# One tile loop for the last two experts of a mixture-of-experts stage, in plain fp32

## The chip, the cores and the metric

The program runs on one core of one Trainium2 chip. The metric is the device time of one execution in microseconds; lower is better. The engines are named as in the profile: PE (TensorE, matrix products; PEld is its weight load), ACT (ScalarE), DVE (VectorE), POOL (GpSimd) and SP (SyncE, which here issues most of the DMAs). PEldq, ACTq and the like are the sequencers of the engines.

## What is computed

Three stages in a row. Block-causal attention (4 batches, 8 heads, 576 rows, 64 columns a head) gives 2304 tokens of 512 columns. A dense layer with 2048 hidden columns and a leaky maximum follows. Then a layer of 8 experts with top-1 routing, around which this case turns:

```python
skip_score = x @ w_skip
do_compute = skip_score > 0
out = x.copy()
xc = x[do_compute]
logits = xc @ w_gate
e_idx = np.argmax(logits, axis=1)
...
for e in range(E):                      # E = 8
    mask = e_idx == e
    if not mask.any():
        continue
    h = np.maximum(xc[mask] @ w1[e], 0.0)      # 512 -> 1024
    y[mask] = gate_w[mask, None] * (h @ w2[e]) # 1024 -> 512
out[do_compute] = xc + y
```

All inputs and outputs are fp32. How many tokens an expert gets depends on the data.

## The kernel before

**The first two stages** (attention, the dense layer's two products in three passes of fp32r each) fill PE until about 610 us and aren't touched, but for one constant: POOL writes a set of tables at the start of the dense layer's second product, each counted by the semaphore `s_tables` (N_TABLES, 20, L470).

**Tiles of the experts.** The tokens of each expert are put in tiles of 128 rows. DVE counts them (L1447 to L1459): the count of each expert plus `fill`, which is 128 (L883), shifted right by 7 bits. Every expert thus has at least one tile, which may be partly or wholly empty. A sum over the experts gives the first tile of each, `base_i`, which every engine loads into registers (`tile_start`, L577; a register load from a tensor, with the register operations after it). One full tile of expert 0, the early tile, is taken from the first tokens already known and is worked through ahead of the loops in straight code, with a second product in plain fp32 (`early_hidden` L1777, `early_y` L1796).

**Eight loops.** PE, ACT and DVE each have eight loops, one for each expert, from that expert's first tile to the next one's; POOL has one over all tiles (L956). What PE does for a tile (L1850 to L1873):

- the first product, 32 products of 128x128 by 128x128 in fp32 (L1859), into the two banks `ps_hid`;
- four transposes of the next tile's rows (L1786);
- the second product, 24 products of 512 columns in fp32r (L1870 to L1872): high by high, high by low and low by high parts, into `ps_y`.

ACT copies the rows (`held`, L1121, then `kept`, L1151), and takes the rectified high part of the hidden values out of `ps_hid` (L1154). DVE takes the low part (L1483), moves the transposed rows (L1463) and multiplies the result by the gate weight and adds the row (L1490). POOL gathers the rows of the tile after next (L941) and scatters the result to the output (L933), both with indirect DMAs.

**Weights.** SP loads 4 MB an expert in eight pieces into four sets of buffers (`w1_sb`, `w2_sb`, `load_expert` L698), expert x into set x mod 4, once the expert four before is done. At the head of an expert's loop, ACT splits off the high part of w2, four pieces of 1024 columns (`high_w2`, L1130), once the last expert's second product is done, since there is one `w2_hi`; DVE makes the low part in place of w2 (`low_w2`, L1468).

Of the kernel before, what the change touches and what calls it, by code (L numbers as in the profile page):

```python
# [7 lines left out]
F32 = mybir.dt.float32  # L8
F32R = mybir.dt.float32r
BF16 = mybir.dt.bfloat16  # L10
I32 = mybir.dt.int32
ALU = mybir.AluOpType
ACT = mybir.ActivationFunctionType
AX = mybir.AxisListType

P = 128
B, H, S, D = 4, 8, 576, 64
N_TOK = B * S
DM = H * D
# [65 lines left out]
MAX_TILES = NT + E  # L85
SKIP = float(1 << 20)
NW = 4


EARLY_BLK = 4  # L90
# [128 lines left out]
def build(nc, q_t, k_t, v_r, w_in, w_out, w_gs, w1, w2, out):  # L219
    ctx = ExitStack()  # L220
    with ctx:
        def sb(name, shape, dt=F32, scope=ctx):
            return scope.enter_context(nc.sbuf_tensor(name, shape, dt))
# [4 lines left out]
        def sem(name):  # L228
            return ctx.enter_context(nc.semaphore(name))
# [106 lines left out]
        sb("gap", [P, max(pad - used, 0) // 4 // 16 * 16 + 16])  # L336


        w1_sb += [sb(f"w1_sb{i}", [P, KC, F]) for i in range(2, NW)]
        w2_sb += [sb(f"w2_sb{i}", [P, EC, DM], F32, raw) for i in range(2, NW)]  # L340
        raw.close()
        w2_lo += [sb(f"w2_lo{i}", [P, EC, DM], F32R) for i in range(2, NW)]
        idx = sb("idx", [P, E * SLOTS], I32)
        below = sb("below", [P, E + 1, E])
        rows = sb("rows", [P, ROW_W])
        held = sb("held", [P, ROW_W])
        kept = sb("kept", [P, ROW_W])
# [86 lines left out]
        s_rank = sem("s_rank")  # L434
        s_tab = sem("s_tab")
        s_cnt = sem("s_cnt")
        s_t = sem("s_t")
        s_early = sem("s_early")
        s_earlyat = sem("s_earlyat")
# [27 lines left out]
        block = ctx.enter_context(nc.Block())  # L467

        N_FULL, N_CONST, N_GAP = 3, 12, 6
        N_TABLES = 20  # L470
        W_LOADS = KC + EC // 2


# [82 lines left out]
        def loaded_to(e, x, n):  # L556

            for k, loaded in enumerate(s_w[x % NW]):
                e.wait_ge(loaded, 16 * (W_LOADS // 2 * (x // NW) + (n + 2 - k) // 2))

        def tab_of(m):

# [69 lines left out]
        def _(e):  # L632
# [133 lines left out]
            for x in range(2, E):  # L766
                if x >= NW:
                    e.wait_ge(s_expert, x - NW + 1)
                    e.wait_ge(s_w2lo, W2_PIECES * (x - NW + 1))
                for n in range(W_LOADS):  # L770
                    load_expert(x, n)
            e.wait_ge(s_count, 1)
            total_tiles = e.value_load(base_i[0:1, E:E + 1], min_val=0, max_val=MAX_TILES)
            for i in range(2):
# [6 lines left out]
        def _(e):  # L781
# [103 lines left out]
            for c in range(KC):  # L885
# [7 lines left out]
            e.tensor_copy(rev[:, :], rev_i[:, :]).then_inc(s_tables, 1)  # L893
            e.affine_select(out=lower[:, :, :], in_=lower[:, :, :], compare_op=ALU.is_gt, fill=0.0,
                            base=0, pattern=[[1, E + 1], [-1, E]], channel_multiplier=0).then_inc(s_tables, 1)


            for ring in range(ACT_RING):
# [71 lines left out]
        def _(e):  # L970
# [148 lines left out]
            def hold(g):  # L1119
                e.wait_ge(m_gather, (g + 1) * 16)  # L1120
                e.copy(held[:, :], rows[:, :]).then_inc(m_held, 1)  # L1121
# [20 lines left out]
            early_relu(1)  # L1142
            starts = tile_starts(e)
            hold(0)
            for x in range(E):
                for n in range(W2_PIECES):
                    high_w2(x, n)
                with e.Fori(starts[x], starts[x + 1]) as g:
                    e.wait_ge(m_held, g + 1)
                    e.wait_ge(m_out, g + 1)  # L1150
                    e.copy(kept[:, :], held[:, :]).then_inc(m_kept, 1)  # L1151
                    for half in range(2):
                        e.wait_ge(m_hid, 2 * g + half + 2)
                        e.activation(hid_hi[:, EC // 2 * half:EC // 2 * (half + 1), :].rearrange("p f c -> p (f c)"),  # L1154
                                     ps_hid[half][:, :], ACT.Relu).then_inc(m_high, 1)
                    e.wait_ge(m_kept, g + 2)
                    hold(g + 1)


        @block.vector  # L1160
        def _(e):
# [296 lines left out]
            e.wait_ge(s_t, 5)  # L1458
            e.tensor_copy(base_i[:, :], base_f[:, :]).then_inc(s_count, 1)  # L1459

            def move_rows_t(g):
                e.wait_ge(m_rt, g + 1)
                e.tensor_copy(rows_t[:, :, :].rearrange("p k c -> p (k c)"), ps_rt[:, :]).then_inc(m_rows, 1)  # L1463

            def low_w2(x, n):
# [7 lines left out]
            e.wait_ge(m_y, 1)  # L1473
            e.scalar_tensor_tensor(out=y_out[:, :], in0=ps_y[:, :], scalar=early[:, DM:DM + 1],
                                   in1=early[:, 0:DM], op0=ALU.mult, op1=ALU.add).then_inc(m_out, 1)
            for x in range(E):
                for n in range(W2_PIECES):
                    low_w2(x, n)
                with e.Fori(starts[x], starts[x + 1]) as g:
                    for half in range(2):  # L1480
                        fs = slice(EC // 2 * half, EC // 2 * (half + 1))
                        e.wait_ge(m_high, 2 * g + half + 2)
                        e.scalar_tensor_tensor(out=hid_lo[:, fs, :].rearrange("p f c -> p (f c)"), in0=ps_hid[half][:, :],  # L1483
                                               scalar=0.0, in1=hid_hi[:, fs, :].rearrange("p f c -> p (f c)").bitcast(F32),
                                               op0=ALU.max, op1=ALU.subtract).then_inc(m_low, 1)
                    move_rows_t(g + 1)
                    e.wait_ge(m_y, g + 2)
                    e.wait_ge(m_kept, g + 2)
                    e.wait_ge(m_scatter, (g + 1) * 16)
                    e.scalar_tensor_tensor(out=y_out[:, :], in0=ps_y[:, :], scalar=kept[:, DM:DM + 1],  # L1490
                                           in1=kept[:, 0:DM], op0=ALU.mult, op1=ALU.add).then_inc(m_out, 1)


        @block.tensor
        def _(e):
# [351 lines left out]
                starts.append(tile_start(e, f))  # L1847
            starts.append(tile_start(e, E))

            for x in range(E):  # L1850
                i = x % NW
                with e.Fori(starts[x], starts[x + 1]) as g:
                    e.wait_ge(m_rows, g + 1)
                    loaded_to(e, x, KC - 1)
                    e.wait_ge(m_low, 2 * g + 1)
                    for half in range(2):
                        for f in range(EC // 2 * half, EC // 2 * (half + 1)):
                            for c in range(KC):
                                last = e.matmul(ps_hid[half][:, P * f - HALF * half:P * (f + 1) - HALF * half],  # L1859
                                                w1_sb[i][:, c, P * f:P * f + P], rows_t[:, c, :],  # L1860
                                                start=c == 0, stop=c == KC - 1)
                        last.then_inc(m_hid, 1)
                    transpose_rows(g + 1)
                    e.wait_ge(m_out, g + 1)
                    for f in range(EC):
                        if f % 2 == 0:
                            e.wait_ge(s_w2lo, W2_PIECES * x + f // 2 + 1)
                        if f % (EC // 2) == 0:
                            e.wait_ge(m_low, 2 * g + f // (EC // 2) + 2)
                        e.matmul(ps_y[:, :], hid_hi[:, f, :], w2_hi[:, f, :], start=f == 0, stop=False)  # L1870
                        e.matmul(ps_y[:, :], hid_hi[:, f, :], w2_lo[i][:, f, :], start=False, stop=False)  # L1871
                        last = e.matmul(ps_y[:, :], hid_lo[:, f, :], w2_hi[:, f, :], start=False, stop=f == EC - 1)  # L1872
                    last.then_inc(m_y, 1)  # L1873


_NAMES = ("q_t", "k_t", "v_r", "w_in", "w_out", "w_gs", "w1", "w2")
# [24 lines left out]
```

## Time and profile before

| | us |
|---|---|
| median of 3 runs (779.55 to 780.79) | 780.35 |
| the profiled execution, its own time | 779.68 |
| span of its instructions in the trace | 777.9 |
| PE busy in that span | 759.8 |
| DVE, ACT, POOL busy | 371.2, 304.2, 151.1 |

The span goes from the first to the last instruction that the profiler recorded, and the 1.78 us between it and the execution's time lie outside the records. Sums below are made against the profiled execution. In the trace a plain fp32 product leaves two records on PE, an fp32r product leaves one. Matmuls are pipelined, so that the duration of one is longer than its distance from the next: the time that a stretch of them takes is read from the chain of waits, not from a mean.

### The profile page before, as it was taken

To read this page: it belongs to the slowest core of one execution; us is meant where nothing else is said; L and a number is where in the kernel's file an instruction comes from. 1 tells how busy PE (TensorE), PEld (TensorE's weight loads), DVE (VectorE), ACT (ScalarE), POOL (GpSimd) and SP (SyncE) were. 2 spreads that over 40 slices of the span, in tenths; PEclk is the share of its full clock that TensorE was granted. 3 is DMA by queue.
4 is the path that set the end of the run, shared out by engine and by line. 5 is a ranking of instruction groups with operands and counts; after the bars stand their busy time and mean duration, and the time that the engine had idled before them with its cause. 6 is when DMAs were issued, how large, how long until landed. Compare 5 with 4: busy or idle time off the path is not lost.

```text
span 777.9 us, 13549 instructions
## 1 busy us (share of the span) xinstructions
PE 759.8 (98%) x4738; PEld 643.7 (83%) x4738; DVE 371.2 (48%) x772; ACT 304.2 (39%) x711; POOL 151.1 (19%) x193
## 2 busy tenths in 40 slices
PE   7999999999999999999999999999999999999997
PEld 4556888888888887999988888888878779898996
DVE  5767455533433563023254556556463341444644
ACT  5566664544344553334432222213221131333533
POOL 3226664312212331100020000000000031222222
PEclk9999999999999999999999999999999999999999
DMA  4336777544544542466665665655552147777750
GB/s 133 118 112 175 206 202 213 159 110 130 150 110 128 148 117 64 139 179 174 182 198 166 184 177 149 191 165 169 165 165 69 37 131 244 234 241 218 241 160 4
DMA packets 97959, 121.68 MB, mean 156 GB/s; under 512 B 14258, under 2 KB 61122, under 8 KB 97896
## 3 DMA queue, kind: packets, MB, share of 16 engines
q1 hardware_dynamic: 94920, 116.50, 51.5%
q0 software_dynamic: 2080, 3.77, 1.5%
q8 instruction: 36, 0.59, 0.3%
q10 hardware_dynamic: 896, 0.59, 0.2%
q14 instruction: 27, 0.22, 0.1%
HBM read 89.35 MB, written 31.57 MB: 155 GB/s over the span
## 4 chain that ended last, share of the span: by engine, by line
PE 91%; ACT 2%; issue 2%; SPq 2%; DMA 2%; DVE 1%; POOL 0%; POOLq 0%; DVEq 0%; ACTq 0%
PE ps_hid L1859 10%; PE ps_h L1615 9%; PE ps_x L1692 9%; PE ps_x L1694 8%; PE ps_x L1693 8%; PE ps_h L1617 8%; PE ps_h L1616 8%; PE ps_o L1597 5%; PE ps_t L1571 4%; PE ps_y L1871 3%; PE ps_y L1872 3%; PE ps_y L1870 3%; PE ps_s L1558 1%; PE ps_s L1559 1%; PE ps_s L1522 1%
## 5 line engine op out<-in xcount | busy, mean ns | idle before, releaser
L1615 PE MATMUL ps_h<-xh,win_h 128*128 128x384 f32 x384 | 135.2, 352 | 3.0 <-ACT act L1013 2.1
L1617 PE MATMUL ps_h<-xh,win_l 128*128 128x384 f32 x384 | 128.7, 335 | 0.0
L1616 PE MATMUL ps_h<-xl,win_h 128*128 128x384 f32 x384 | 128.7, 335 | 0.0
L1692 PE MATMUL ps_x<-wout_h,g_hi 128*128 128x512 f32 x288 | 114.6, 398 | 0.0
L1694 PE MATMUL ps_x<-wout_h,g_lo 128*128 128x512 f32 x288 | 112.4, 390 | 0.0
L1693 PE MATMUL ps_x<-wout_l,g_hi 128*128 128x512 f32 x288 | 112.2, 389 | 0.0
L1013 ACT ACTIVATE act<-ps_h 128x384 f32<-128x384 f32 x96 | 47.2, 491 | 149.0 <-PE ps_h L1617 148.7
L1194 DVE TENSOR_REDUCE neg_max<-ps_s 128x1 f32<-128x128 f32 (+3 forms) x144 | 71.0, 509 | 48.8 <-PE ps_s L1559 26.5
L999 ACT ACTIVATE prob<-ps_s,neg_max 128x128 f32<-128x128 f32 (+3 forms) x144 | 78.9, 550 | 37.8 <-DVE neg_max L1194 30.6
L1859 PEld LDWEIGHTS ps_hid<-rows_t,w_sb 128*128 128x128 f32 x704 | 80.2, 192 | 1.7 <-issue 0.8
L1615 PEld LDWEIGHTS ps_h<-xh,win_h 128*128 128x128 f32 x384 | 72.1, 188 | 11.6 <-ACT act L1013 5.8
L1234 DVE TENSOR_TENSOR g_lo<-g_raw,g_hi 128x512 fp32r<-128x512 f32 x72 | 49.6, 689 | 65.8 <-ACT g_hi L1023 65.3
L1859 PE MATMUL ps_hid<-rows_t,w_sb 128*128 128x128 f32 x704 | 80.5, 275 | 0.0
L1616 PEld LDWEIGHTS ps_h<-xl,win_h 128*128 128x128 f32 x384 | 72.3, 188 | 0.0
L1617 PEld LDWEIGHTS ps_h<-xh,win_l 128*128 128x128 f32 x384 | 72.1, 188 | 0.0
L1200 DVE COPY pt<-ps_t 128x384 f32<-128x384 f32 (+4 forms) x113 | 46.8, 434 | 51.9 <-PE ps_t L1571 51.6
L1692 PEld LDWEIGHTS ps_x<-wout_h,g_hi 128*128 128x128 f32 x288 | 54.1, 188 | 12.3 <-issue 2.0
L1694 PEld LDWEIGHTS ps_x<-wout_h,g_lo 128*128 128x128 f32 x288 | 54.1, 188 | 11.6
L1693 PEld LDWEIGHTS ps_x<-wout_l,g_hi 128*128 128x128 f32 x288 | 54.1, 188 | 10.4
L1023 ACT ACTIVATE g_hi<-g_raw 128x512 fp32r<-128x512 f32 x72 | 43.8, 630 | 47.1 <-DVE g_raw L1229 31.7
L1229 DVE SCALAR_TENSOR_TENSOR g_raw<-g_raw 128x512 f32<-128x512 f32 x72 | 49.3, 686 | 15.9 <-DMA g_raw<-hidden 15.6
L1571 PE MATMUL ps_t<-ident,prob 128*128 128x128 f32 x339 | 54.8, 278 | 0.9 <-DVE pt L1200 0.7
(187 smaller groups left out, 1064.0 us busy)
## 6 DMA issues: line engine op xcount, KB each, us to landing
w_sb<-in_w SPq DMA_DIRECT2D x64, 512.0 KB, 5.3
hidden<-act SPq DMA_DIRECT2D x96, 192.0 KB, 2.3
g_raw<-hidden SPq DMA_DIRECT2D x72, 256.0 KB, 4.3
k_raw<-in_k_t SPq DMA_DIRECT2D x40, 144.0 KB, 3.0
x2rows<-x SPq DMA_DIRECT2D x18, 256.0 KB, 2.4
out<-x SPq DMA_DIRECT2D x18, 256.0 KB, 2.7
w_stage<-in_w_in SPq DMA_DIRECT2D x16, 256.0 KB, 3.1
w_stage<-in_w_out SPq DMA_DIRECT2D x16, 256.0 KB, 3.0
```

The source lines that it names most:

```text
L999: e.activation(prob_of(u), score_out(u), ACT.Exp, bias=neg_max[:, u % 4:u % 4 + 1], scale=1.0, accum_out=row_sum[p % 2][:, sum_column(u):s ...
L1194: e.tensor_reduce(out=neg_max[:, u % 4:u % 4 + 1], in_=src, axis=AX.XY if u % UNITS == TAIL else AX.X, op=ALU.max, negate=True).then_inc(s ...
L1229: e.scalar_tensor_tensor(out=raw[:, :, :], in0=raw[:, :, :], scalar=0.01, in1=raw[:, :, :], op0=ALU.mult, op1=ALU.max).then_inc(s_leaky, 1)
L1234: e.tensor_tensor(g_lo[j % G_RING][:, :, :], g_raw[j % RAW_RING][:, :, :], g_hi[j % G_RING][:, :, :].bitcast(F32), ALU.subtract).then_inc( ...
L1571: last = e.transpose(t_bank(u, P, P * kt, P * kt + P), tile[:, P * kt:P * kt + P], ident[:, :])
L1615: e.matmul(dst, win_h[:, f, kc, :], xh[slot][:, kc, :], start=kc == 0, stop=False)
L1616: e.matmul(dst, win_h[:, f, kc, :], xl[slot][:, kc, :], start=False, stop=False)
L1617: last = e.matmul(dst, win_l[:, f, kc, :], xh[slot][:, kc, :], start=False, stop=kc == KC - 1)
L1692: e.matmul(dst, hi, wout_h[:, f, :], start=f == 0, stop=False)
L1693: e.matmul(dst, hi, wout_l[:, f, :], start=False, stop=False)
L1694: last = e.matmul(dst, lo, wout_h[:, f, :], start=False, stop=f == FC - 1)
L1859: last = e.matmul(ps_hid[half][:, P * f - HALF * half:P * (f + 1) - HALF * half], w1_sb[i][:, c, P * f:P * f + P], rows_t[:, c, :], start= ...
```

## The change

Experts 6 and 7 (SHARED is 6, the first of them) get one loop on PE, ACT and DVE, from the first tile of expert 6 to the end. Their weights lie in two-part tensors, `w1_two` and `w2_two`, in the places of sets 2 and 3. DVE makes a table `second_i`, which holds for each tile whether it is of expert 7, and PE and ACT load the entry of each tile into a register.

In the shared loop ACT copies the tile's w1, chosen by that register, in two halves into `w1_sb[0]`, the set of expert 4, and PE's first product reads it there. The second product is 8 products in plain fp32 whose moving operand is `w2_two`, addressed by the register; w2 of these two experts isn't split. The hidden values are rectified in fp32, the first half by ACT, the second by DVE, into `hid_early`. The entry of `fill` of the last expert is 127 in place of 128. SP waits for the last load before its end.

```diff
--- before.py
+++ after.py
@@ -85,6 +85,8 @@
 MAX_TILES = NT + E
 SKIP = float(1 << 20)
 NW = 4
+
+SHARED = E - 2
 
 
 EARLY_BLK = 4
@@ -336,12 +338,16 @@
         sb("gap", [P, max(pad - used, 0) // 4 // 16 * 16 + 16])
 
 
-        w1_sb += [sb(f"w1_sb{i}", [P, KC, F]) for i in range(2, NW)]
-        w2_sb += [sb(f"w2_sb{i}", [P, EC, DM], F32, raw) for i in range(2, NW)]
+        w1_two = sb("w1_two", [P, 2, KC, F])
+        w1_sb += [w1_two[:, i, :, :] for i in range(2)]
+        w2_two = sb("w2_two", [P, 2, EC, DM], F32, raw)
+        w2_sb += [w2_two[:, i, :, :] for i in range(2)]
         raw.close()
         w2_lo += [sb(f"w2_lo{i}", [P, EC, DM], F32R) for i in range(2, NW)]
         idx = sb("idx", [P, E * SLOTS], I32)
         below = sb("below", [P, E + 1, E])
+        second_f = sb("second_f", [P, MAX_TILES])
+        second_i = sb("second_i", [P, MAX_TILES], I32)
         rows = sb("rows", [P, ROW_W])
         held = sb("held", [P, ROW_W])
         kept = sb("kept", [P, ROW_W])
@@ -434,6 +440,8 @@
         s_rank = sem("s_rank")
         s_tab = sem("s_tab")
         s_cnt = sem("s_cnt")
+        s_second = sem("s_second")
+        m_shared = sem("m_shared")
         s_t = sem("s_t")
         s_early = sem("s_early")
         s_earlyat = sem("s_earlyat")
@@ -467,7 +475,7 @@
         block = ctx.enter_context(nc.Block())
 
         N_FULL, N_CONST, N_GAP = 3, 12, 6
-        N_TABLES = 20
+        N_TABLES = 21
         W_LOADS = KC + EC // 2
 
 
@@ -557,6 +565,11 @@
 
             for k, loaded in enumerate(s_w[x % NW]):
                 e.wait_ge(loaded, 16 * (W_LOADS // 2 * (x // NW) + (n + 2 - k) // 2))
+
+        def loaded_second(e, second, n):
+
+            for k, loaded in enumerate(s_w[(E - 1) % NW]):
+                e.wait_ge(loaded, second * (16 * ((n + 2 - k) // 2)) + 16 * (W_LOADS // 2))
 
         def tab_of(m):
 
@@ -769,6 +782,7 @@
                     e.wait_ge(s_w2lo, W2_PIECES * (x - NW + 1))
                 for n in range(W_LOADS):
                     load_expert(x, n)
+            loaded_to(e, E - 1, W_LOADS - 1)
             e.wait_ge(s_count, 1)
             total_tiles = e.value_load(base_i[0:1, E:E + 1], min_val=0, max_val=MAX_TILES)
             for i in range(2):
@@ -893,6 +907,8 @@
             e.tensor_copy(rev[:, :], rev_i[:, :]).then_inc(s_tables, 1)
             e.affine_select(out=lower[:, :, :], in_=lower[:, :, :], compare_op=ALU.is_gt, fill=0.0,
                             base=0, pattern=[[1, E + 1], [-1, E]], channel_multiplier=0).then_inc(s_tables, 1)
+
+            e.memset(fill[:, E - 1:E], float(P - 1)).then_inc(s_tables, 1)
 
 
             for ring in range(ACT_RING):
@@ -1142,7 +1158,7 @@
             early_relu(1)
             starts = tile_starts(e)
             hold(0)
-            for x in range(E):
+            for x in range(SHARED):
                 for n in range(W2_PIECES):
                     high_w2(x, n)
                 with e.Fori(starts[x], starts[x + 1]) as g:
@@ -1155,6 +1171,28 @@
                                      ps_hid[half][:, :], ACT.Relu).then_inc(m_high, 1)
                     e.wait_ge(m_kept, g + 2)
                     hold(g + 1)
+
+                    e.sem_inc(m_shared, 2)
+
+            e.wait_ge(s_second, 2)
+            loaded_to(e, SHARED, KC - 1)
+            with e.Fori(starts[SHARED], starts[E]) as g:
+                second = e.value_load(second_i[0:1, bass.ds(g, 1)], min_val=0, max_val=1)
+                e.wait_ge(m_hid, 2 * g + 1)
+                loaded_second(e, second, KC - 1)
+                e.sem_inc(s_carry, 1)
+                for half in range(2):
+                    e.copy(w1_sb[0][:, :, HALF * half:HALF * half + HALF],
+                           w1_two[:, bass.ds(second, 1), :, HALF * half:HALF * half + HALF].rearrange(
+                               "p o k f -> p (o k) f")).then_inc(m_shared, 1)
+                e.wait_ge(m_held, g + 1)
+                e.wait_ge(m_out, g + 1)
+                e.copy(kept[:, :], held[:, :]).then_inc(m_kept, 1)
+                e.wait_ge(m_hid, 2 * g + 2)
+                e.activation(hid_early[:, 0:EC // 2, :].rearrange("p f c -> p (f c)"), ps_hid[0][:, :],
+                             ACT.Relu).then_inc(m_high, 2)
+                e.wait_ge(m_kept, g + 2)
+                hold(g + 1)
 
 
         @block.vector
@@ -1458,6 +1496,10 @@
             e.wait_ge(s_t, 5)
             e.tensor_copy(base_i[:, :], base_f[:, :]).then_inc(s_count, 1)
 
+            e.tensor_scalar(second_f[:, :], iota_f[:, 0:MAX_TILES], base_f[:, E - 1:E], None, ALU.is_ge).then_inc(s_second, 1)
+            e.wait_ge(s_second, 1)
+            e.tensor_copy(second_i[:, :], second_f[:, :]).then_inc(s_second, 1)
+
             def move_rows_t(g):
                 e.wait_ge(m_rt, g + 1)
                 e.tensor_copy(rows_t[:, :, :].rearrange("p k c -> p (k c)"), ps_rt[:, :]).then_inc(m_rows, 1)
@@ -1473,7 +1515,7 @@
             e.wait_ge(m_y, 1)
             e.scalar_tensor_tensor(out=y_out[:, :], in0=ps_y[:, :], scalar=early[:, DM:DM + 1],
                                    in1=early[:, 0:DM], op0=ALU.mult, op1=ALU.add).then_inc(m_out, 1)
-            for x in range(E):
+            for x in range(SHARED):
                 for n in range(W2_PIECES):
                     low_w2(x, n)
                 with e.Fori(starts[x], starts[x + 1]) as g:
@@ -1489,6 +1531,16 @@
                     e.wait_ge(m_scatter, (g + 1) * 16)
                     e.scalar_tensor_tensor(out=y_out[:, :], in0=ps_y[:, :], scalar=kept[:, DM:DM + 1],
                                            in1=kept[:, 0:DM], op0=ALU.mult, op1=ALU.add).then_inc(m_out, 1)
+            with e.Fori(starts[SHARED], starts[E]) as g:
+                e.wait_ge(m_hid, 2 * g + 3)
+                e.tensor_scalar(hid_early[:, EC // 2:EC, :].rearrange("p f c -> p (f c)"), ps_hid[1][:, :], 0.0, None,
+                                ALU.max).then_inc(m_low, 2)
+                move_rows_t(g + 1)
+                e.wait_ge(m_y, g + 2)
+                e.wait_ge(m_kept, g + 2)
+                e.wait_ge(m_scatter, (g + 1) * 16)
+                e.scalar_tensor_tensor(out=y_out[:, :], in0=ps_y[:, :], scalar=kept[:, DM:DM + 1],
+                                       in1=kept[:, 0:DM], op0=ALU.mult, op1=ALU.add).then_inc(m_out, 1)
 
 
         @block.tensor
@@ -1847,7 +1899,7 @@
                 starts.append(tile_start(e, f))
             starts.append(tile_start(e, E))
 
-            for x in range(E):
+            for x in range(SHARED):
                 i = x % NW
                 with e.Fori(starts[x], starts[x + 1]) as g:
                     e.wait_ge(m_rows, g + 1)
@@ -1873,6 +1925,33 @@
                     last.then_inc(m_y, 1)
 
 
+            loaded_to(e, SHARED, W_LOADS - 1)
+            e.wait_ge(s_second, 2)
+            with e.Fori(starts[SHARED], starts[E]) as g:
+                second = e.value_load(second_i[0:1, bass.ds(g, 1)], min_val=0, max_val=1)
+                e.wait_ge(m_rows, g + 1)
+                e.wait_ge(m_high, 2 * g + 1)
+                e.wait_ge(m_low, 2 * g + 1)
+                for half in range(2):
+                    e.wait_ge(m_shared, 2 * g + half + 1)
+                    for f in range(EC // 2 * half, EC // 2 * (half + 1)):
+                        for c in range(KC):
+                            last = e.matmul(ps_hid[half][:, P * f - HALF * half:P * (f + 1) - HALF * half],
+                                            w1_sb[0][:, c, P * f:P * f + P], rows_t[:, c, :],
+                                            start=c == 0, stop=c == KC - 1)
+                    last.then_inc(m_hid, 1)
+                transpose_rows(g + 1)
+                e.wait_ge(m_out, g + 1)
+                loaded_second(e, second, W_LOADS - 1)
+                e.wait_ge(m_high, 2 * g + 3)
+                for f in range(EC):
+                    if f == EC // 2:
+                        e.wait_ge(m_low, 2 * g + 3)
+                    last = e.matmul(ps_y[:, :], hid_early[:, f, :], w2_two[:, bass.ds(second, 1), f, :],
+                                    start=f == 0, stop=f == EC - 1)
+                last.then_inc(m_y, 1)
+
+
 _NAMES = ("q_t", "k_t", "v_r", "w_in", "w_out", "w_gs", "w1", "w2")
```

## Rows read from the trace of the kernel before

**Rows 1.** The page's busy shares and granted clock, 40 slices of the whole span:
```profile
PE 759.8 (98%) x4738; PEld 643.7 (83%) x4738; DVE 371.2 (48%) x772; ACT 304.2 (39%) x711; POOL 151.1 (19%) x193
...
PEclk9999999999999999999999999999999999999999
```

**Rows 2.** Chain of waits, last two tiles: start us, us, what held the chain:
```profile
740.35 0.44 PE ps_rt L1786 x4
...
746.34 7.14 PE ps_hid L1859 x64
753.48 0.44 PE ps_rt L1786 x4
...
759.49 7.14 PE ps_hid L1859 x64
...
767.07 0.23 PE ps_y L1870
...
772.65 0.03 issue
...
772.78 0.76 DVE y_out L1490
...
774.44 1.03 POOL out L933
```

**Rows 3.** Groups by line, whole span: the first product of the tile loops:
```profile
L1859 PE MATMUL ps_hid<-rows_t,w_sb 128*128 128x128 f32 x704 | 80.5, 275 | 0.0
```

**Rows 4.** The last scatter, window 774 to 777.9 us: its queue, its landing:
```profile
q0 software_dynamic: 80, 0.00, 1.0%
...
out<-y_out,scatter_at POOLq DMA_INDIRECT x1, 2.1
```

**Rows 5.** The scatter before it, window 761 to 765.5 us: the same lines:
```profile
q0 software_dynamic: 80, 0.05, 3.8%
...
out<-y_out,scatter_at POOLq DMA_INDIRECT x1, 2.9
```

**Rows 6.** Chain of waits, the early tile, whose second product is plain fp32:
```profile
620.60 0.46 issue
621.05 5.41 PE ps_y L1796 x12
...
626.90 0.86 PE ps_y L1796 x2
```

**Rows 7.** Timeline of ACT, 738 to 755 us: start, us, line, operation, idle before:
```profile
740.88 0.62 ACT L1121 COPY held<-rows 128x516 f32<-128x516 f32 x1
746.53 3.90 ACT L1130 ACTIVATE w_hi<-w_sb 128x1024 fp32r<-128x1024 f32 x4 [5.04 <-PE ps_y L1872]
750.34 0.61 ACT L1151 COPY kept<-held 128x516 f32<-128x516 f32 x1
...
753.52 0.60 ACT L1154 ACTIVATE hid_hi<-ps_hid 128x512 fp32r<-128x512 f32 x1 [2.08 <-PE ps_hid L1859]
```

**Rows 8.** Register loads of the tile starts (line L577), min/median/max ns:
```profile
L577 ACTq TENSOR_LOAD <-base_i x9: 272/275/478, 620.2 to 624.7; - x9
...
L577 PEldq TENSOR_LOAD <-base_i x9: 295/307/496, 620.2 to 625.9; - x9
L577 ACTq FUSED_REGOPS  x9: 147/147/178, 620.7 to 625.0; - x9
```

**Rows 9.** PE's own sequencer at the loop head L1852, 745 to 773 us:
```profile
L1852 PEldq COMPARE_BRANCH  x2: 70/70/70, 755.3 to 768.4; - x2
```

**Rows 10.** Timeline of DVE around the count of the tiles:
```profile
619.97 0.17 DVE L1459 CAST base_i<-base_f 128x9 int32<-128x9 f32 x1
626.94 0.69 DVE L1463 COPY rows_t<-ps_rt 128x512 f32<-128x512 f32 x1 [6.79 <-PE ps_rt L1786]
```

**Rows 11.** SP's last seven weight loads, 729.5 to 748 us: issue ns, start, landing:
```profile
L698 SPq DMA_DIRECT2D w_sb<-in_w x7: 327/328/434, 729.5 to 747.2; - x7
...
DMA to landing us min/median/max: 4.3/5.1/8.5
```

## The prediction

> **What bounds the kernel now.** I read the page's busy shares first. PE is busy for 98% of the span, and its granted clock is in the top tenth in every slice, the level of 2.4 GHz [rows 1]. So a change pays only if it takes work from PE or shortens what comes behind PE's last product. Then I read the end of the chain of waits. It shows one tile as PE sees it: 7.14 us for the first product, 0.44 for four transposes, and the rest, from 767.07 to 772.65 (5.58 us), for the second product of 24 fp32r products, 0.23 us apart [rows 2]. One tile follows the next without a gap: 746.34 to 759.49 is 13.15 us, and 759.49 to 772.65 is 13.16. Behind the last product come DVE's 0.76 us, POOL's scatter, and its landing: 777.9 - 772.65 = 5.25 us of tail.
>
> **How many tiles there are.** The first product has 704 records, 64 a tile [rows 3], so the loops ran 704 / 64 = 11 times. The reference, computed with its own inputs, gives the experts 466, 26, 180, 67, 72, 79, 26 and 0 tokens. With 128 of expert 0 taken early, (count + 128) shifted by 7 gives 3, 1, 2, 1, 1, 1, 1 and 1 tiles, which is 11 as well. The eleventh is expert 7's, with no token. The trace agrees: the last scatter moved 0.00 MB [rows 4], the one before it 0.05 MB, that is expert 6's 26 rows of 2 KB [rows 5]. So the tile at 759.49 to 772.65 does nothing for the output, at full price.
>
> **What the change removes.** With 127 in the last entry, (0 + 127) shifted by 7 is 0: expert 7 has no tile, and the shared loop runs once, for expert 6. PE loses the stretch from 759.49 to 772.65: -13.16 us. Nothing covers it, since PE was the chain. The splits of w2 also go for experts 6 and 7. Those of expert 6, 3.90 us on ACT [rows 7] with DVE's part beside it, lie beside PE's first product and are worth nothing in themselves; had the first product not covered them, each would have cost its whole length.
>
> **What it adds on PE.** The second product of expert 6 is now 8 plain fp32 products. The early tile has the same: 12 records in 5.41 us, and the last 2, one product, in 0.86 us [rows 6]. 8 x 0.86 = 6.88 us against 5.58: +1.30 us. By the 12 records it would be 16 x 0.451 = 7.2, but six register loads sit between those, so I take 0.86; the other figure would add 0.3.
>
> **The register on PE.** A value load costs PE's sequencer 0.31 us, and the register operations behind it 0.15 by ACT's row [rows 8]: 0.46 in all, and exactly that is the one hole of 0.46 us where PE stood for a count that had only just come [rows 6]. In the loop the sequencer is ahead: it passed the loop head at 755.3, when the array reached it only at 759.49 [rows 2, 9], 4.2 us later. That lead covers 0.46 us, so I take 0; without it the cost would be 0.46. A product with its address from a register is nowhere on PE in this trace. Its bounds are 0 (the address is ready while the product before it runs, 0.86 us) and 0.15 us for each of 8, 1.2 us; I take 0, for the six register loads in the early tile were also hidden behind fp32 products.
>
> **The new wait: w1 through ACT.** ACT can start to copy once it has held tile 9's rows, at 740.88 + 0.62 = 741.50 [rows 7], by which time PE has left the first product of the tile before (740.35 [rows 2]). A register load adds 0.44, so 741.9. A half is 2048 columns. Four pieces of 1024 took 3.90 us [rows 7], so two halves take at most 3.90: the first is there at about 743.9, the second at 745.8. PE wants the first at 746.34 and the second half-way through the first product, at 749.9. Slack is 2.4 and 4.1 us; cost 0. Behind the copies on ACT wait `kept`, which needs the result of the tile before (after 747 us, so it isn't delayed), and the first half's maximum, wanted at 749.9, when ACT is free. DVE's half of the maximum starts at 753.5 and is wanted after four fp32 products, 3.4 us into the second product. The weights must have landed: the last seven loads are expert 7's and start at 729.5, so expert 6's eight are issued before, and at the longest landing of 8.5 us [rows 11] are there by 738.
>
> **Small things.** DVE's two operations that make the table come behind the tile count [rows 10] and take about 0.2 us each. DVE then loads nine registers and waits for PE's transposes until 626.94; its loads end near 626.0, so 0.4 us are just hidden. If not, PE's first tile comes late by 0 to 0.3 us; I take 0. POOL's extra memset lies in the dense stage, 200 us before it is wanted. The increments on ACT in the other loops are 0. SP's new wait is for expert 7's last load, issued at 747.2 and landed by 755.7 at worst [rows 11], before the new end.
>
> **The tail.** Before, the last scatter was the empty one and landed after 2.1 us [rows 4]. Now it is expert 6's, with 26 rows; in this trace, on quiet queues, it took 2.9 [rows 5]. So +0.8 us.
> The Trainium skill, "DMA: Bandwidth & Descriptors", section "Anatomy of one DMA — SWDGE (gpsimd) path", gives about 2.0 us plus bytes over 436 KB per us; by it, as an estimate, 53 KB cost 0.1 us more than none, and the sum would be 0.7 us lower.
>
> **The sum.** -13.16 + 1.30 + 0.8 = -11.06 us. The profiled execution of 779.68 becomes 768.6. The median of the runs shown lies 0.67 above the profiled one, so 780.35 - 11.06 = 769.3; with 0.1 for the small things, **769.4**.
>
> **Rivals.**
> *The shared loop starts late.* ACT's copies are a new producer ahead of PE's first product. For it: they begin only after `held`, and neither the copy by register nor the code of this loop has a row. Against it: 2.4 us of slack. If the copies took twice as long (7.8 us), the first half would come at 745.8, still in time, and the second at 749.7, just in time; so it must come from a late start of 4 to 5 us, the length of a whole weight load [rows 11], and then costs PE about 2 to 3: 772.
> The Trainium skill, "Runtime: NRT & Kernel Launch", section "Instruction fetch mechanics", says that a taken branch to code that isn't loaded stalls until a DMA has brought it, which is such a late start; the branches of PE's loop head in this trace took 70 ns [rows 9] and show none.
> *Register-addressed products cost PE its lead.* If each of the 16 records waited for the sequencer (0.46 us each [rows 8] in place of being ahead), the second product would be 7.4 us longer: 776.8. It would undo the gain only from 11.06 / 8 = 1.4 us a product.
> *The empty tile stays* (the change doesn't do what it says, or the data of the timed runs give expert 7 tokens). Then both tiles have fp32 second products and nothing goes: 780.35 + 2 x 1.30 = 783.0, slower. It decides as soon as expert 7 has one token. Against it: rows 3 and rows 4 fit zero tokens.
>
> **How the numbers follow.** Forecast 0.83, late start 0.09, lost lead 0.04, empty tile stays 0.04. The range must hold 8 in 10: below, the last scatter at the price of the empty one (-0.8, rows 4) and the runs' distance from lowest to median (0.8) give 767.8; above, the bounds of the unknown costs (0.3 + 0.46 + 1.2) and most of the late start give 772.3. Faster by over 0.2% (1.6 us, about what a measurement of this kernel can tell from no change): 0.95, the forecast, the late start and nearly all of the lost lead. Within: 0.01, the far end of the lost lead. Slower: 0.04.
>
> **What would show it.** In the profile after: 640 records of first product in loops; nothing of w2's splits for experts 6 and 7 (24 of ACT's 32 pieces left); the last first product at 746.3 without idle time before it; 16 fp32 records of 512 columns in 6.9 us; PE's last product at about 760.8; the end 6 us later, at 766.8. Idle time of PE ahead of the last first product, put down to ACT's copy, would be the late start; a second product over 8 us the lost lead; 704 records the empty tile.

## The result and the profile after

The changed kernel takes 767.71 us (median of 4 runs, 767.56 to 768.32) against 779.95 before (4 runs, 778.81 to 780.79): 12.24 us less, a ratio of 0.9845 with a 95% interval of 0.9828 to 0.9862. The forecast was 769.4, in a range from 767.8 to 772.3: the measured median lies 1.7 below the forecast and 0.1 below the lower end of the range. The forecast set 769.4 against a median of 780.35 of three runs; a fourth has brought that median to 779.95. As a ratio the forecast is 0.9860, which lies in the interval.

The page of the changed kernel opens with these lines, which answer to [rows 1]:

```profile
PE 747.9 (98%) x4638; PEld 630.3 (82%) x4639; DVE 359.5 (47%) x761; ACT 297.3 (39%) x701; POOL 147.3 (19%) x190
...
PEclk9999999999999999999999999999999999999999
```

PE is still the engine that sets the time, at the same clock, with 11.9 us less to do; the span went from 777.9 to 765.9. The chain of waits of its end, whose lines answer to [rows 2] (start, duration, what held the chain):

```profile
740.04 0.44 PE ps_rt L1838 x4
...
746.03 7.14 PE ps_hid L1939 x64
753.17 0.44 PE ps_rt L1838 x4
753.61 6.88 PE ps_y L1950 x16
760.49 0.03 issue
...
760.62 0.76 DVE y_out L1542
...
762.28 1.03 POOL out L949
```

There is one tile fewer. The last one begins at 746.03 with no hole before it and takes 14.46 us, up to 760.49: 7.14 for the first product, 0.44 for the transposes, 6.88 for the plain fp32 product. The tail behind it is 765.9 - 760.49 = 5.41 us. The timeline of ACT in the same stretch answers to [rows 7]:

```profile
740.57 0.61 ACT L1137 COPY held<-rows 128x516 f32<-128x516 f32 x1
741.59 3.71 ACT L1185 COPY w_sb<-w_two 128x2048 f32 x2 [0.40 <-DMA w_two<-in_w]
747.02 0.62 ACT L1190 COPY kept<-held 128x516 f32<-128x516 f32 x1 [1.73 <-DVE y_out L1532]
749.70 0.60 ACT L1192 ACTIVATE hid_early<-ps_hid 128x512 f32<-128x512 f32 x1 [2.06 <-PE ps_hid L1939]
```

The two copies of w1 run from 741.59 to 745.30, and both are done before PE starts at 746.03. The 0.40 us before them are put down to a weight load, but expert 6's w1 was there long before: SP issues a piece only when the piece two before it has landed, so its last piece of w1 had landed when the sixth of the eight loads was issued, at 724.6. Nor are the 0.40 us the register load. That ran on ACT's sequencer from 740.7 to 741.2, beside the copy of `held` (740.57 to 741.18); behind it came the register operations of the next wait and of the copy's addresses (L572 and L1185, 741.2 to 741.6). The forecast reckoned 0.44 us behind `held`, nearly the same length for another reason. DVE's two new operations stand behind the count of the tiles, and its first `rows_t` is still released by PE ([rows 10] before, a wait of 6.79 us there):

```profile
619.80 0.23 DVE L1499 TENSOR_SCALAR second_f<-iota_f,base_f 128x26 f32<-128x26 f32 x1
620.07 0.18 DVE L1501 CAST second_i<-second_f 128x26 int32<-128x26 f32 x1
626.68 0.69 DVE L1505 COPY rows_t<-ps_rt 128x512 f32<-128x512 f32 x1 [6.43 <-PE ps_rt L1838]
```

The stretch ahead of the loops varies between executions of the same kernel: two more profiles of the changed kernel (the runs `e0_after` and `e11_after` below) begin the last tile at 746.07 and 747.28. So below, a kernel is judged in its trace by two differences that don't contain that stretch: from the start of a tile's first product to the end of its second, and from there to the end of the span.

The experiments ran in four groups, each beside the kernel before on the same chip. Its medians there were 779.37 (e0, e1, e5, e7), 779.95 (e2, e3, e4), 780.61 (e8 to e11) and 780.78 us (e12). The changed kernel was timed again in two of them:

> The changed kernel once more, as the yardstick for the three that run beside it. Expected 767.7 us, as in its first runs, against 779.9 before; one loop tile less on PE (13.16 us), a second product 1.30 us longer.

Measured: 768.03 us (4 runs, 767.25 to 768.72), ratio 0.9855 (0.984 to 0.987).

> The changed kernel again, beside the three others: 767.7 us.

Measured: 768.88 us (5 runs, 767.97 to 769.70), ratio 0.9849 (0.9835 to 0.9862). A difference of 1 us between groups is thus nothing; only kernels of one group are compared by their times.

### The profile page after: what moved, and what is told of

Its sections match the earlier page's. It is cut to its first block, busy times and chain, and to the rows that moved or that the text cites. A ratio compares the mean times of both kernels' runs of the same rounds, so it can differ in the third digit from the quotient of the medians.

```text
span 765.9 us, 13309 instructions
## 1 busy us (share of the span) xinstructions
PE 747.9 (98%) x4638; PEld 630.3 (82%) x4639; DVE 359.5 (47%) x761; ACT 297.3 (39%) x701; POOL 147.3 (19%) x190
## 4 chain that ended last, share of the span: by engine, by line
PE 94%; ACT 2%; issue 2%; DVE 1%; DMA 0%; POOL 0%; DVEq 0%; POOLq 0%; ACTq 0%
PE ps_h L1667 10%; PE ps_x L1744 9%; PE ps_h L1669 9%; PE ps_x L1746 9%; PE ps_h L1668 9%; PE ps_x L1745 9%; PE ps_hid L1911 8%; PE ps_o L1649 6%; PE ps_t L1623 4%; PE ps_y L1923 2%; PE ps_y L1924 2%; PE ps_y L1922 2%; PE ps_s L1574 2%; PE ps_s L1610 2%; PE ps_s L1611 1%
## 5 line engine op out<-in xcount | busy, mean ns | idle before, releaser
L1649 PE MATMUL ps_o<-pt,v_sb 128*64 128x320 f32 (+4 forms) x448 | 51.7, 365 | 1.1 <-ACT pt L1060 0.6
L1623 PEld LDWEIGHTS ps_t<-ident,prob 128*128 128x128 f32 x339 | 39.9, 141 | 11.5 <-issue 4.8
```

The lines of the kernel that those rows point to most:

```text
L1623: last = e.transpose(t_bank(u, P, P * kt, P * kt + P), tile[:, P * kt:P * kt + P], ident[:, :])
L1649: last = e.matmul(ps_o[own, a:a + cols], v_sb[p % 2][:, kt, own], pt[p % 2][:, h, at:at + cols], start=kt == 0, stop=kt == tiles - 1)
```

## Experiments: the entry of 127 alone

The edit, on the kernel before:

```diff
-        N_TABLES = 20
+        N_TABLES = 21
...
+            e.memset(fill[:, E - 1:E], float(P - 1)).then_inc(s_tables, 1)
...
+            loaded_to(e, E - 1, W_LOADS - 1)
```

> The kernel before with one part of the change alone: 127 for 128 in the last entry of fill (and SP's wait for the last weight load). Theory (all of the gain is the missing tile): PE's last product ends 13.16 us earlier, near 759.5 minus what the start differs; the splits of w2 for expert 7 are still made on ACT and DVE, from that moment on, and end about 5.8 us later (0.2 to ACT's start, 3.9, then 1.6 for DVE's last piece), which is about when the scatter has landed. The scatter is issued while DVE splits, so it takes 1.6 us to issue in place of 1.0 and lands 0.6 later: a tail 0.2 to 0.8 longer than the 5.25 of before. So 766.9 to 767.7 us: at least as fast as the changed kernel, although two of its three parts are missing. Rival (the shared loop or the fp32 product itself brings part of the gain): 768.5 or more.

Measured: 774.93 us (5 runs, 774.60 to 775.50), ratio 0.9943 (0.993 to 0.9957). That is 4.4 us below the kernel before, and over 7 above the theory's 767.7. The rival had set no upper end (768.5 or more), but its reason isn't what happened either. The tile isn't missing. The end of its chain of waits:

```profile
758.62 7.14 PE ps_hid L1861 x64
765.76 0.44 PE ps_rt L1788 x4
...
771.53 0.25 PE ps_y L1874
771.78 0.03 issue
...
771.91 0.75 DVE y_out L1492
```

PE did an eleventh tile. The sequencers tell why. First the loop of PE (L1854), then that of POOL (L958); min/median/max ns, first and last start in us:

```profile
L1854 PEldq COMPARE_BRANCH  x11: 67/70/249, 636.2 to 767.6; - x11
L1854 PEldq MOVE  x8: 37/37/38, 625.7 to 754.5; - x8
```

```profile
L958 POOLq COMPARE_BRANCH  x10: 40/45/55, 642.0 to 760.2; - x10
L958 POOLq MOVE  x1: 29/29/29, 629.1 to 629.1; - x1
```

POOL loops from 0 to the number of tiles and did 10 rounds, so the count was 10 and expert 7 began and ended at 10. PE has 8 MOVEs, one for each loop it entered, but 11 rounds (704 records of its first product, 64 a round) and 11 branches: one branch at the foot of each round and none at a loop's head. **The body of such a loop ran once with equal bounds.** What this kernel gained is nearly all in its tail: POOL has no result of an eleventh tile to scatter, so behind PE's last product only 772.9 - 771.78 = 1.1 us are left in place of 5.25.

The second run of this kind asked for the same missing tile with a guard around the splits of w2 (`last_i` is min(tiles of expert 7, 1), made by DVE):

```diff
+                    with e.Fori(0, e.value_load(last_i[0:1, 0:1], min_val=0, max_val=1)):
+                        for n in range(W2_PIECES):
+                            high_w2(x, n)
```

> The kernel before with 127 in the last entry of fill, its eight loops and three-pass products kept, and the splits of w2 for expert 7 inside a loop of as many rounds as min(tiles of expert 7, 1), which is right for any data. Theory: PE ends as in the run with fill alone; no split runs beside the last scatter, so it issues in 1.03 us and lands in 2.3, tail 5.4. 779.9 - 13.16 + 0.2 = 767.0 us (766.5 to 767.3), 0.7 to 1.1 less than the changed kernel, for the plain fp32 product (1.30 longer) is avoided. Rival (a register load and a second loop cost ACT or DVE more than the cover): 767.7 or more.

Measured: 774.92 us (5 runs, 773.67 to 775.46), ratio 0.9939 (0.9926 to 0.9953), again with a tile too many. It ran in the same group as the first, and its guard shows the same a second time. Its bound is min(tiles of expert 7, 1), which is 0 by the count above, and its body ran once: ACT still made all 32 pieces, the last four at 759.85.

```profile
L1134 ACT ACTIVATE w_hi<-w_sb x32: 1039/1042/1057, 625.9 to 762.7; 128x1024 fp32r<-128x1024 f32 x32
```

So neither part of the change can drop the tile alone. The entry of 127 makes it empty of rounds; the shared loop, which always has expert 6's tile to begin with, is what lets PE, ACT and DVE skip it.

## Experiments: the shared loop alone, and its price

The changed kernel with 128 in all entries (the added memset taken out, N_TABLES back to 20):

> The changed kernel with 128 in all entries of fill: the shared loop runs for expert 6's tile and for expert 7's empty one. Theory: nothing is removed and two second products are 1.30 us longer each: 779.9 + 2.6 = 782.5 us (782.0 to 783.0), slower than before; in the second round ACT's copy starts after held of that tile and has 6.88 us of PE's second product as its cover, so no hole. Rival (the loop itself saves time, or its copy stalls the second round): below 781.5, or above 784 with PE idle before the last first product.

Measured: 782.34 us (5 runs, 781.91 to 784.26), ratio 1.0034 (1.0021 to 1.0048): slower than before by 2.4, where 2.6 was reckoned. Both rounds of the shared loop stand in its chain of waits:

```profile
746.01 7.14 PE ps_hid L1938 x64
753.16 0.44 PE ps_rt L1837 x4
...
760.47 7.14 PE ps_hid L1938 x64
767.61 0.44 PE ps_rt L1837 x4
768.05 6.88 PE ps_y L1949 x16
```

760.47 - 746.01 = 14.46 us a round, 1.31 more than a three-pass tile, and no hole in the second round either, whose copy had to wait for `held` of the first. The tail behind it, with a last scatter of no rows, is 780.2 - 774.93 = 5.27 us.

Next, the changed kernel without copy and registers:

```diff
-                second = e.value_load(second_i[0:1, bass.ds(g, 1)], min_val=0, max_val=1)
...
-                                            w1_sb[0][:, c, P * f:P * f + P], rows_t[:, c, :],
+                                            w1_sb[SHARED % NW][:, c, P * f:P * f + P], rows_t[:, c, :],
...
-                    last = e.matmul(ps_y[:, :], hid_early[:, f, :], w2_two[:, bass.ds(second, 1), f, :],
+                    last = e.matmul(ps_y[:, :], hid_early[:, f, :], w2_sb[SHARED % NW][:, f, :],
```

> The changed kernel without its registers: the shared loop reads expert 6's w1 and w2 at fixed addresses, with no copy of w1 through ACT and no load of a register (it would be wrong for tiles of expert 7, of which there are none in these inputs). Theory (copy, register load and register addresses are all covered): the same time as the changed kernel within 0.3 us. Rival (register addressing costs PE time): faster by up to 1.2 us, 16 records in less than 6.88 us.

Measured: 767.69 us (4 runs, 767.37 to 768.55) beside 768.03 (767.25 to 768.72) for the changed kernel, a difference well inside both spreads. Its last tile:

```profile
745.65 7.14 PE ps_hid L1929 x64
752.79 0.44 PE ps_rt L1830 x4
753.23 6.88 PE ps_y L1939 x16
```

753.23 + 6.88 - 745.65 = 14.46 us, the same to a hundredth. Copy, register load and register address cost PE nothing.

How much cover was left was measured with the copy made longer, each half copied first to a free set (twice), and to a second one (three times):

```diff
+                    e.copy(w1_sb[1][:, :, HALF * half:HALF * half + HALF], src)
+                    e.copy(w2_sb[0][:, KC * half:KC * half + KC, :], src)
                     e.copy(w1_sb[0][:, :, HALF * half:HALF * half + HALF], src).then_inc(m_shared, 1)
```

> The changed kernel with each half of w1 copied twice by ACT, first to a set that is free, then to its place: the halves are ready 1.86 and 3.71 us later. From the trace of the changed kernel: copies start at 741.59, so the first half is there at 745.3, wanted at 746.03; the second at 749.0, wanted at 749.6. Theory (slack of 2.6 and 4.3 us): no change, 767.7 within 0.3 us. Rival (slack smaller than read): 0.5 to 2 us slower, PE idle before its last first product.

Measured: 767.65 us (5 runs, 766.52 to 769.73), ratio 0.9842 (0.9827 to 0.9857): no change. The copies took 741.51 to 748.82 in its timeline, and PE had no hole.

> The changed kernel with each half copied three times: first half at 747.2 (1.1 us late), second at 752.7, which is 3.1 us after the 749.6 at which PE wants it. Theory: 3.1 us slower than the changed kernel, 770.8 us (770.4 to 771.3), with PE idle 1.1 us before and 2.0 us in the last first product. Rival (the copies are not on PE's path): no change.

Measured: 771.36 us (4 runs, 770.42 to 772.14), 3.7 above the one before it. The timeline of PE, with its idle time in brackets:

```profile
746.73 3.81 PE L1940 MATMUL ps_hid<-rows_t,w_sb 128*128 128x128 f32 x32 [1.20 <-ACT w_sb L1188]
752.03 3.84 PE L1940 MATMUL ps_hid<-rows_t,w_sb 128*128 128x128 f32 x32 [1.50 <-ACT w_sb L1188]
```

Both halves are now late, each put down to ACT's last copy of the half. Against the time at which `held` started (740.07 here, 740.57 in the changed kernel), PE's last product ends at 763.19 - 740.07 = 23.12 us in place of 760.49 - 740.57 = 19.92: 3.2 us, where 3.1 was expected. (The brackets add up to 2.7; the rest is that each half, started afresh, takes 3.81 and 3.84 us in place of 7.14 / 2 = 3.57.) So the copies are truly ahead of PE, and their slack is more than their own length.

## Experiments: a version without the plain fp32 product

If the shared loop is needed for the empty tile and the fp32 product is a loss, the shared loop can keep the three passes: ACT splits w2 by register for each tile, and PE reads fixed places. The core of the edit:

```diff
+                e.wait_ge(m_y, g + 1)
+                for n in range(W2_PIECES):
+                    e.copy(w2_hi[:, 2 * n:2 * n + 2, :],
+                           w2_two[:, bass.ds(second, 1), 2 * n:2 * n + 2, :].rearrange(
+                               "p o k f -> p (o k) f")).then_inc(m_w2h, 1)
...
+                    e.tensor_tensor(w2_lo[0][:, 2 * n:2 * n + 2, :],
+                                    w2_two[:, bass.ds(second, 1), 2 * n:2 * n + 2, :].rearrange("p o k f -> p (o k) f"),
+                                    w2_hi[:, 2 * n:2 * n + 2, :].bitcast(F32), ALU.subtract).then_inc(m_w2l, 1)
```

> The shared loop with the three-pass second product kept: for each tile ACT copies w1 by register as in the changed kernel, then splits off the high part of w2 by register (four pieces), DVE writes the low part to the free set of expert 4; PE reads fixed addresses. Theory (the loop has to be shared so that its body, which runs at least once, has a tile to work on; the plain fp32 product was a loss of 1.30 us and the splits lie beside PE's first product, as they did before): 1.30 us less than the changed kernel, 767.7 - 1.3 = 766.4 us (766.0 to 766.9), PE's second product of the last tile back at 5.58 us, and the scatter of the tile before the last, which then has a split beside it, issued in 1.62 us in place of 1.03. Rival (ACT can't do a w1 copy and a split in one tile in time): PE idle in the last tile, 767.5 or more.

Measured: 766.62 us (5 runs, 766.11 to 768.83), ratio 0.9829 (0.9816 to 0.9843), beside the 768.88 of the changed kernel in the same group. The intervals of the two ratios overlap, so the times alone hardly separate the two; the traces do. The chain of waits, and the timeline of ACT:

```profile
746.32 7.14 PE ps_hid L1956 x64
753.47 0.44 PE ps_rt L1859 x4
753.90 0.23 PE ps_y L1967
...
759.47 0.03 issue
```

```profile
741.95 3.71 ACT L1188 COPY w_sb<-w_two 128x2048 f32 x2 [0.47 <-DMA w_two<-in_w]
746.43 3.89 ACT L1193 CAST w_hi<-w_two 128x1024 fp32r x4 [0.78 <-PE ps_y L1945]
750.23 0.62 ACT L1198 COPY kept<-held 128x516 f32<-128x516 f32 x1
750.75 0.59 ACT L1201 ACTIVATE hid_hi<-ps_hid 128x512 fp32r<-128x512 f32 x1
```

The last tile is back at 759.47 - 746.32 = 13.15 us against 14.46. ACT copies w1 beside the second product of the tile before and splits w2 beside the first product, where it did so before, and PE has no hole. Its tail is 764.8 - 759.47 = 5.33 us. By its trace it is the best of all versions, and its code serves tiles of both experts, though these inputs have none of expert 7. Its price is that the split is made again for each tile of the two experts, which this data with one tile can't show.

## Experiments: the last scatter

The tail had come out shorter than forecast. The last scatter moved the same 0.05 MB as in [rows 5], but took POOL 1.03 us to issue in place of 1.62 (shown below) and landed 2.3 us after its start in place of 2.9:

```profile
q0 software_dynamic: 80, 0.05, 2.5%
...
out<-y_out,scatter_at POOLq DMA_INDIRECT x1, 2.3
```

The scatters come in two kinds, and which one is not a matter of rows. From POOL's timeline in the changed kernel, the results of experts 3, 4, 5 and 6:

```profile
721.55 1.64 POOL L949 DMA_INDIRECT out<-y_out,scatter_at  x1 [4.02 <-DVE y_out L1532]
734.69 1.64 POOL L949 DMA_INDIRECT out<-y_out,scatter_at  x1 [4.01 <-DVE y_out L1532]
747.82 1.03 POOL L949 DMA_INDIRECT out<-y_out,scatter_at  x1 [4.01 <-DVE y_out L1532]
762.27 1.03 POOL L949 DMA_INDIRECT out<-y_out,scatter_at  x1 [6.13 <-DVE y_out L1542]
```

The long ones fall in the time in which ACT and DVE split the next expert's w2; with the splits of experts 6 and 7 gone, the last two are short. The kernel before shows the same: a full tile of expert 0 (0.26 MB), whose next tile is of the same expert and needs no split, and the 26 rows of expert 1 and of expert 6 (0.05 MB), with a split beside each:

```profile
643.03 1.03 POOL L933 DMA_INDIRECT out<-y_out,scatter_at  x1 [4.03 <-DVE y_out L1490]
...
682.42 1.61 POOL L933 DMA_INDIRECT out<-y_out,scatter_at  x1 [2.97 <-DVE y_out L1490]
...
761.28 1.62 POOL L933 DMA_INDIRECT out<-y_out,scatter_at  x1 [4.02 <-DVE y_out L1490]
```

Where e8 brought a split back at the place of the last scatter but one, that scatter took 1.83 us. Three runs asked which engine does it, with work that reads and writes free sets, put right behind the last result.

```diff
+                for c in (2, 3):
+                    e.tensor_tensor(w1_sb[1][:, c, :], w1_sb[1][:, 0, :], w1_sb[1][:, 1, :], ALU.subtract)
```

> The changed kernel with two subtractions of 1024 columns on DVE right behind the last result, beside POOL's last scatter. Theory (an indirect DMA takes POOL 1.62 in place of 1.03 us to issue when DVE works on such a two-input operation at that time, and the number of rows has no part in it): the last scatter is issued in about 1.6 us and lands later by as much, 0.6 us slower than the changed kernel. Rival (it is the rows or the position in the loop that count): 1.03 us, no change.

Measured: the scatter was issued in 1.14 us and landed after 2.4; 769.14 us (4 runs, 768.54 to 770.03) beside 768.88. Neither the 1.6 of the theory nor quite the 1.03 of the rival; the times don't differ.

```diff
+                e.wait_ge(m_out, g + 2)
+                for c in (2, 3):
+                    e.copy(w1_sb[1][:, c, :], w1_sb[1][:, 0, :])
```

> The changed kernel with two copies of 1024 columns on ACT behind the last result, beside POOL's last scatter, as control to the same with DVE. Theory (DVE is what slows POOL's issue, not ACT): 1.03 us, the time of the changed kernel within 0.3 us. Rival (any engine beside it): 1.6 us, 0.6 slower.

Measured: 1.03 us, landed after 2.3; 768.72 us (5 runs, 768.01 to 769.82). ACT alone does nothing to it. The last run has both edits at once (ACT's copies now read expert 6's w1 and write another free set):

> The changed kernel with both at once behind the last result: two subtractions of 1024 columns on DVE and two copies of 1024 columns on ACT, beside POOL's last scatter. DVE alone made its issue 1.14 us, ACT alone left it at 1.03, and the scatters of the kernel before that had both beside them took 1.62. Theory (it takes both together): 1.5 to 1.7 us, and the end 0.5 us later behind PE's last product (5.9 in place of 5.4). Rival (the splits' fp32r output or their place in memory counts, not the engines): 1.1 to 1.2 us.

Measured, from its timeline:

```profile
761.46 2.35 DVE L1548 TENSOR_TENSOR w_sb<-w_sb 128x1024 f32<-128x1024 f32 x2
761.57 1.99 ACT L1198 COPY w_sb<-w_two 128x1024 f32<-128x1024 f32 x2 [10.60 <-DVE y_out L1545]
762.43 1.15 POOL L949 DMA_INDIRECT out<-y_out,scatter_at  x1 [6.13 <-DVE y_out L1545]
```

768.73 us (4 runs, 767.97 to 769.11), with 1.15 us for the issue: the rival's figure. The end came 766.1 - 760.65 = 5.45 us behind PE's last product, where the theory had 5.9. The theory that it takes both engines fell. That the long issues come with the splits of w2 is shown by their place in every kernel here. What in the splits does it is open: their fp32r output and where their tensors lie weren't tried, and PE, which ran its first product beside every long issue, was idle beside the scatters of these three runs. (PE alone doesn't do it: it ran beside the issue of 1.03 us at 643.03 as well.)

## Why the prediction was right, point by point

- **What bounds the kernel**: right. PE was the chain to its last product, and what left PE left the time.
- **What is removed** (-13.16): right in size, and incomplete in its reason. The step "with 127 in the last entry, (0 + 127) shifted by 7 is 0: expert 7 has no tile" gave all of it to that entry. The run with the entry alone kept PE's tile, since its loop's body ran once. The tile goes only because expert 7 also shares its loop. The change had both parts, so the forecast held; that it needs both was not foreseen, and that part of the hit is luck. The profile of before could have shown the form of the loops. Over its whole span PE's sequencer has

```profile
L1852 PEldq COMPARE_BRANCH  x11: 67/70/253, 637.0 to 768.4; - x11
L1852 PEldq MOVE  x8: 37/37/38, 626.5 to 755.4; - x8
```

  that is 8 entries, but only one branch for each of the 11 rounds, the first at 637.0. The branch at 755.3 in [rows 9], which the prediction took for the loop's head, is the foot of expert 6's round; the entry into expert 7's loop is the MOVE at 755.4, so the lead of about 4 us stands.
- **The fp32 product** (+1.30): 6.88 us measured, as reckoned from the early tile's pair of 0.86 [rows 6]. The other reading, 7.2, was wrong.
- **Register and address on PE** (0, bounds 0.46 and 1.2): 0. The tile is 14.46 us with and without them.
- **w1 through ACT** (0, slack 2.4 and 4.1): 0. The copies began 0.41 us behind `held`, where 0.44 was reckoned. The halves were ready at about 743.4 and 745.3, 2.6 and 4.3 us early. Doubling the copies cost nothing, tripling them 3.2 us.
- **Small things** (0.1): DVE's 0.41 us stayed behind its wait for PE; nothing was seen of them.
- **The tail** (+0.8): this is the term that was mis-sized. It measured 5.41 - 5.25 = +0.16. The 2.9 us of [rows 5] held 0.6 us of a long issue that went with the splits, which the change removes as well; rows cost only 2.3 - 2.1 = 0.2 us in the landing, and 5.41 - 5.27 = 0.14 against the shared loop with an empty last tile. For the bytes alone the trace about agrees with the estimate of 0.1 by the Trainium skill, "DMA: Bandwidth & Descriptors", section "Anatomy of one DMA — SWDGE (gpsimd) path".
- **The sum**: -13.16 + 1.31 + 0.16 = -11.7 in the trace, and the last tile began 0.3 us earlier (746.03 for 746.34), which is within what that stretch varies: -12.0 of span, where -11.06 was forecast. The 1.7 us between 769.4 and 767.71 are thus 0.64 of the tail, 0.3 of that stretch, 0.67 by which the forecast set the median above the profiled execution (the profiled execution of the changed kernel was its median), and the 0.1 of small things. The lower end of the range had allowed for the tail (0.8) and for the spread of the runs (0.8), and not for the stretch ahead of the loops.
- **The rivals**: no late start, no lost lead. Of the signs named, the records of the first product in loops are 384 + 192 + 64 = 640, 24 of ACT's 32 splits are left, the last first product starts at 746.03 without idle time before it, and PE's last product ends at 760.49; only the end, at 765.9, is earlier than the 766.8 named. The empty tile that stays is real for a change with one part of it left out: 782.34 us with 128 kept, where the rival had 783.0.

## What to carry to other kernels

Before counting on a loop of no rounds, look in the sequencer's rows for a branch at the loop's entry; if, as here, each round has one at its foot and the entry none, a case that may be empty has to share a loop with one that isn't. When a change has several parts, ask which of them carries the gain and which is only a cost that came with it: here the plain fp32 product cost 1.3 us, and the three passes could be kept. And when a price is read from a row, see what else runs beside that row, for the change may take that away too.

## What the runs showed of the hardware that wasn't expected

- The body of a loop with equal bounds ran once, on PE, ACT and DVE alike (11 rounds where POOL's count was 10; 32 pieces made under a guard of 0).
- An indirect scatter took POOL 1.61 to 1.97 us to issue beside the splits of w2 (1.97 is the early tile's, at 630.88 before) and 1.02 to 1.04 otherwise, with 128 rows as with none; beside two-input fp32 work on DVE it took 1.14, beside copies on ACT 1.03, beside both 1.15.
- A plain fp32 product whose moving operand is addressed by a register took the same 0.43 us a record (6.88 us for 16) as one at a fixed address.
